# An attention product folded into two feed-forward layers in fp32: weight product in three fp32r passes, first loads regrouped, small tiles padded to 64 bytes

## What is computed

```python
qn = q / (norm(q, axis=1) + 1e-06)      # q, k, v: (1, 6016, 256)
kn = k / (norm(k, axis=1) + 1e-06)
s = kn.transpose(0, 2, 1) @ qn / tau    # (256, 256)
s = s - s.max(-1, keepdims=True)
a = exp(s); a /= a.sum(-1, keepdims=True) + 1e-09
x = v @ a
h = x @ w_in                            # (256, 2048)
x = (h - tanh(h)) @ w_out               # (2048, 256)
h = x @ w_in2
g = where(h > 0, h, exp(min(h, 0)) - 1)
out = g @ w_out2
```

## Time and profile before

| | |
|---|---|
| median of 3 runs (lowest, highest) | 1108.56 us (1108.1, 1110.02) |
| the profiled execution: its time, its span | 1108.33 us, 1106.5 us |
| PE busy | 1097.6 us, 99% of the span, 4892 matmul records |
| DVE, ACT, POOL busy | 703.6 (64%), 533.3 (48%), 0.8 us (0%) |
| chain that ended last | PE 98%, DVE 1%, DMA 1% |
| DMA | 33.42 MB; 344 and 333 GB/s in the first two of 40 slices, 1 to 20 in most later ones |

### The profile page before, as it was taken

How to read it: one execution, slowest core, us unless ns; L and a number is a source line. 1 busy time by engine, 2 the same in 40 slices (tenths; PEclk the granted TensorE clock), 3 DMA queues, 4 the chain that set the end, 5 groups by cost and what they waited for, 6 DMA issues and landing times.

```text
span 1106.5 us, 14123 instructions
## 1 busy us (share of the span) xinstructions
PE 1097.6 (99%) x4892; PEld 904.8 (82%) x4892; DVE 703.6 (64%) x1133; ACT 533.3 (48%) x891; POOL 0.8 (0%) x7
## 2 busy tenths in 40 slices
PE   8999999999999999999999999999999999999998
PEld 7768888888888888888888888888888888888998
DVE  5676666665665656666666666666565565666565
ACT  6565555444444544544544444444454444444443
POOL 0000000000000000000000000000000000000000
PEclk9999999999999999999999999999999999999999
DMA  9941010110101101001011011010110010001010
GB/s 344 333 112 20 1 20 1 20 19 1 20 1 20 19 0 19 12 7 19 0 19 19 0 19 19 0 19 3 16 19 0 14 19 0 0 4 16 1 20 15
DMA packets 105710, 33.42 MB, mean 30 GB/s; under 512 B 96849, under 2 KB 101841, under 8 KB 105169
## 3 DMA queue, kind: packets, MB, share of 16 engines
q1 hardware_dynamic: 105680, 33.04, 12.1%
HBM read 26.87 MB, written 6.16 MB: 30 GB/s over the span
## 4 chain that ended last, share of the span: by engine, by line
PE 98%; DVE 1%; DMA 1%; ACT 0%; SPq 0%; issue 0%; ACTq 0%
PE h_ps L356 16%; PE h_ps L358 15%; PE h_ps L357 15%; PE x_ps L358 8%; PE x_ps L356 8%; PE out_ps L358 8%; PE out_ps L356 8%; PE x_ps L357 8%; PE out_ps L357 8%; PE x_ps L364 3%; PE out_ps L414 1%; DMA q_ring<-q_dram 1%; PE h_ps L414 0%; PE x_ps L414 0%; DVE g_lo L675 0%; SPq L288 0%
## 5 line engine op out<-in xcount | busy, mean ns | idle before, releaser
L675 DVE TENSOR_TENSOR g_lo<-g,g_hi 128x512 fp32r<-128x512 f32 (+1 forms) x384 | 261.4, 681 | 225.3 <-ACT g_hi L616 116.8
L616 ACT ACTIVATE g_hi<-g 128x512 fp32r<-128x512 f32 (+1 forms) x192 | 119.6, 623 | 205.6 <-DVE g L793 205.2
L602 ACT ACTIVATE g_hi<-g 128x512 fp32r<-128x512 f32 (+1 forms) x192 | 119.6, 623 | 131.3 <-PE x_ps L358 70.5
L609 ACT ACTIVATE g<-h_ps 128x512 f32<-128x512 f32 (+1 forms) x192 | 113.1, 589 | 142.2 <-PE h_ps L358 141.4
L774 DVE TENSOR_TENSOR g<-h_ps,g 128x512 f32<-128x512 f32 (+1 forms) x192 | 129.6, 675 | 34.6 <-ACT g L595 34.5
L356 PE MATMUL h_ps<-x_hi,w_in_hi 128*128 128x512 f32 (+1 forms) x384 | 149.6, 390 | 0.1
L356 PE MATMUL h_ps<-vT_hi,wf_hi 128*128 128x512 f32 (+1 forms) x384 | 149.6, 390 | 0.0
L357 PE MATMUL h_ps<-vT_lo,wf_hi 128*128 128x512 f32 (+1 forms) x384 | 149.5, 389 | 0.0
L358 PE MATMUL h_ps<-x_hi,w_in_lo 128*128 128x512 f32 (+1 forms) x384 | 149.2, 389 | 0.0
L789 DVE TENSOR_SCALAR g<-g 128x512 f32<-128x512 f32 (+1 forms) x192 | 80.9, 421 | 107.4 <-ACT g L609 106.4
L358 PE MATMUL x_ps<-g_hi,w_out_lo 128*128 128x512 f32 (+1 forms) x384 | 149.0, 388 | 0.0
(11 more groups left out here) (90 smaller groups left out, 1080.3 us busy)
## 6 DMA issues: line engine op xcount, KB each, us to landing
v_blocks<-v_dram SPq DMA_DIRECT2D x88, 64.0 KB, 2.2
out_dram<-out_sb SPq DMA_DIRECT2D x88, 64.0 KB, 1.9
k_ring<-k_dram SPq DMA_DIRECT2D x9, 512.0 KB, 9.7
q_ring<-q_dram SPq DMA_DIRECT2D x9, 512.0 KB, 10.2
stage_a<-moe_w_in_dram SPq DMA_DIRECT2D x1, 2048.0 KB, 10.2
stage_b<-moe_w_out_dram SPq DMA_DIRECT2D x1, 2048.0 KB, 9.5
w_in_raw<-moe_w_in_dram SPq DMA_DIRECT2D x1, 2048.0 KB, 9.1
stage_a<-moe_w_out_dram SPq DMA_DIRECT2D x1, 2048.0 KB, 8.2
```

The source lines that it names most:

```text
L602: nc.scalar.activation(g1_hi[i % 2][:, 0:n], g1[i % 2][:, 0:n], ACT.Copy).then_inc(g1_rounded, 1)
L609: nc.scalar.activation(g2[i % 2][:, 0:n], h2_ps[i % 2][:, 0:n], ACT.Exp).then_inc(exp2_ready, 1)
L616: nc.scalar.activation(g2_hi[i % 2][:, 0:n], g2[i % 2][:, 0:n], ACT.Copy).then_inc(g2_rounded, 1)
L675: return nc.vector.tensor_tensor(lo, x, hi.bitcast(F32), ALU.subtract)
```

## The change

1. `CHUNKS` begins with 2, 2, 3 rows in place of 1, 1, 2, 3; there are 14 chunks in place of 15. `DIRECT` is 2. The q transfers of the first three chunks are issued by ACT, ahead of everything else on its queue; SP issues the k transfers and the rest. The load of tau moves behind the seventh chunk.
2. w_in is loaded in four transfers of 512 KB, one for each g. ACT rounds each into `w_in1_hi`, DVE forms the rest into `w_in1_lo`, in place over `stage_a`. `w_in1_hi` lies over the ring buffers that are last used by chunks 8 and 9. ACT writes `aT_hi` in place of `aT`, and DVE forms `aT_lo`. Each of the eight parts of the weight product is six fp32r matmuls (high-high, high-low, low-high, two each) in place of two plain fp32 ones.
3. The nine small tiles take 64 bytes each, so that all tiles start on multiples of 64.

```diff
-CHUNKS = [1, 1, 2, 3] + [4] * 9 + [2, 2]
+CHUNKS = [2, 2, 3] + [4] * 9 + [2, 2]
-DIRECT = 3
+DIRECT = 2
+Q_BESIDE = 3
 TAIL = 4
+FREED_FIRST = [i % RING for i in (LAST - TAIL - 1, LAST - TAIL)]
+ALIGNED = 16
...
-        stage_a = sb("stage_a", [P, CC * F])
+        with ExitStack() as early:
+            stage_a = sb("stage_a", [P, CC * F], stack=early)
+        w_in1_lo = sb("w_in1_lo", [P, GROUPS, CC, 512], F32R)
...
-        aT = sb("aT", [P, CC, C])
-        tau_sb, inv_tau = sb("tau_sb", [P, 1]), sb("inv_tau", [P, 1])
...
+        aT_hi, aT_lo = sb("aT_hi", [P, CC, C], F32R), sb("aT_lo", [P, CC, C], F32R)
+        def column(name, n):
+            return sb(name, [P, ALIGNED])[:, 0:n]
+        tau_sb, inv_tau = column("tau_sb", 1), column("inv_tau", 1)
...
         with ExitStack() as early:
-            k_ring = [sb(f"k_ring{i}", [P, CH, C], stack=early) for i in range(RING)]
...
+            k_ring = {i: sb(f"k_ring{i}", [P, CH, C], stack=early) for i in FREED_FIRST}
...
         with ExitStack() as early:
+            w_in1_hi = sb("w_in1_hi", [P, GROUPS, CC, 512], F32R, stack=early)
...
                 for ring, rows_of, loaded in ((k_ring, k_rows, loaded_k), (q_ring, q_rows, loaded_q)):
-                    sp.dma_start(ring[i % RING][:, 0:rows, :],
-                                 rows_of[:, ROW0[i]:ROW0[i] + rows, :]).then_inc(loaded[i % RING], 16)
-                if i == 0:
+                    if ring is k_ring or i >= Q_BESIDE:
+                        sp.dma_start(ring[i % RING][:, 0:rows, :],
+                                     rows_of[:, ROW0[i]:ROW0[i] + rows, :]).then_inc(loaded[i % RING], 16)
+                if i == RING:
                     sp.dma_start(tau_sb[:, :], tau.rearrange("(a b) -> a b", a=1).to_broadcast([P, 1])).then_inc(loaded_tau, 16)
-            sp.dma_start(stage_a[:, :].rearrange("p (a f) -> p a f", a=CC),
-                         w_in1.rearrange("(a p) f -> p a f", p=P)).then_inc(loaded_w_in1, 16)
+            w_in1_rows = w_in1.rearrange("(a p) f -> p a f", p=P)
+            for g in range(GROUPS):
+                sp.dma_start(stage_a[:, g * CC * 512:(g + 1) * CC * 512].rearrange("p (a f) -> p a f", a=CC),
+                             w_in1_rows[:, :, g * 512:(g + 1) * 512]).then_inc(loaded_w_in1[g], 16)
...
             for n, (g, m) in enumerate(WF_ORDER):
+                rows = slice(m * P, (m + 1) * P)
                 pe.wait_ge(aT_ready[m], 1)
+                pe.wait_ge(w_in1_rounded, g + 1)
                 if n in (4, 5):
                     pe.wait_ge(wf_split, n - 3)
                 for d in range(CC):
-                    last = nc.tensor.matmul(wf_ps[n][:, :], aT[:, d, m * P:(m + 1) * P],
-                                            w_in1_sb[:, d, g * 512:(g + 1) * 512], start=d == 0, stop=d == CC - 1)
+                    nc.tensor.matmul(wf_ps[n][:, :], aT_hi[:, d, rows], w_in1_hi[:, g, d, :], start=d == 0, stop=False)
+                pe.wait_ge(w_in1_split, g + 1)
+                for d in range(CC):
+                    nc.tensor.matmul(wf_ps[n][:, :], aT_hi[:, d, rows], w_in1_lo[:, g, d, :], start=False, stop=False)
+                pe.wait_ge(aT_split[m], 1)
+                for d in range(CC):
+                    last = nc.tensor.matmul(wf_ps[n][:, :], aT_lo[:, d, rows], w_in1_hi[:, g, d, :], start=False, stop=d == CC - 1)
                 last.then_inc(wf_multiplied, 1)
...
         @block.scalar
         def _(act):
+            q_rows = q[0].rearrange("(p r) c -> p r c", p=P)
+            for i in range(Q_BESIDE):
+                act.dma_start(q_ring[i][:, 0:CHUNKS[i], :], q_rows[:, ROW0[i]:ROW0[i] + CHUNKS[i], :]).then_inc(loaded_q[i], 16)
             act.wait_ge(ones_ready, 1)
...
+            def round_w_in1(g):
+                act.wait_ge(loaded_w_in1[g], 16)
+                if g == 0:
+                    act.wait_ge(chunk_multiplied, LAST - TAIL + 1)
+                nc.scalar.activation(w_in1_hi[:, g, :, :], stage_a[:, g * CC * 512:(g + 1) * CC * 512].rearrange("p (a f) -> p a f", a=CC),
+                                     ACT.Copy).then_inc(w_in1_rounded, 1)
+            for g in range(GROUPS - 1):
+                round_w_in1(g)
             act.wait_ge(norms_ready, 1)
             nc.scalar.activation(root[:, :], norms_ps[:, 0:2 * CC], ACT.Sqrt).then_inc(rooted, 1)
             nc.scalar.activation(table_warm[:, 1:2], ones[:, 0:1], ACT.Exp)
+            round_w_in1(GROUPS - 1)
...
-                nc.scalar.activation(aT[:, :, m * P:(m + 1) * P], aT_ps[m][:, 0:C].rearrange("p (d c) -> p d c", d=CC),
+                nc.scalar.activation(aT_hi[:, :, m * P:(m + 1) * P], aT_ps[m][:, 0:C].rearrange("p (d c) -> p d c", d=CC),
                                      ACT.Copy).then_inc(aT_ready[m], 1)
...
+            def split_w_in1(g):
+                dve.wait_ge(w_in1_rounded, g + 1)
+                minus(w_in1_lo[:, g, :, :], stage_a[:, g * CC * 512:(g + 1) * CC * 512].rearrange("p (a f) -> p a f", a=CC),
+                      w_in1_hi[:, g, :, :]).then_inc(w_in1_split, 1)
...
             norm_steps = [0]
+            split_w_in1(0)
             dve.wait_ge(rooted, 1)
...
             norm_step(nc.vector.tensor_scalar(rk[:, :], inv_norm[:, CC:2 * CC], inv_tau[:, 0:1], None, ALU.mult))
+            split_w_in1(1)
             dve.wait_ge(rq_ready, 1)
             for m in range(CC):
+                if m == 1:
+                    split_w_in1(2)
                 dve.wait_ge(scores_ready, m + 1)
...
+            def split_aT(m):
+                dve.wait_ge(aT_ready[m], 1)
+                rows = slice(m * P, (m + 1) * P)
+                minus(aT_lo[:, :, rows], aT_ps[m][:, 0:C].rearrange("p (d c) -> p d c", d=CC), aT_hi[:, :, rows]).then_inc(aT_split[m], 1)
+            split_aT(0)
+            split_w_in1(3)
             for m in range(CC):
                 dve.wait_ge(exp_ready, m + 1)
...
             for cc in range(CC):
                 transpose_v(0, cc)
+            split_aT(1)
             split_wf(0)
```

More of the change, by code:

```diff
@@ L118, in attention_ffn_kernel @@
         g1_lo = [sb(f"g1_lo{i}", [P, TILE], F32R) for i in range(2)]
-        stage_a = sb("stage_a", [P, CC * F])
+        with ExitStack() as early:
+            stage_a = sb("stage_a", [P, CC * F], stack=early)
+        w_in1_lo = sb("w_in1_lo", [P, GROUPS, CC, 512], F32R)
         ident = sb("ident", [P, P])
         ones = sb("ones", [P, P])
-        aT = sb("aT", [P, CC, C])
-        tau_sb, inv_tau = sb("tau_sb", [P, 1]), sb("inv_tau", [P, 1])
[L124 to L128, removed]
-        with ExitStack() as early:
-            k_ring = [sb(f"k_ring{i}", [P, CH, C], stack=early) for i in range(RING)]
-            q_ring = [sb(f"q_ring{i}", [P, CH, C], stack=early) for i in range(RING)]
+        aT_hi, aT_lo = sb("aT_hi", [P, CC, C], F32R), sb("aT_lo", [P, CC, C], F32R)
+        def column(name, n):
+            return sb(name, [P, ALIGNED])[:, 0:n]
+        tau_sb, inv_tau = column("tau_sb", 1), column("inv_tau", 1)
+        root, inv_norm = column("root", 2 * CC), column("inv_norm", 2 * CC)
+        rk = column("rk", CC)
+        table_warm = column("table_warm", 2)
+        neg_max = column("neg_max", CC)
+        row_sum, inv_sum = column("row_sum", CC), column("inv_sum", CC)
+        with ExitStack() as early:
+            k_ring = {i: sb(f"k_ring{i}", [P, CH, C], stack=early) for i in FREED_FIRST}
+            q_ring = {i: sb(f"q_ring{i}", [P, CH, C], stack=early) for i in FREED_FIRST}
+            for i in range(RING):
+                if i not in FREED_FIRST:
+                    k_ring[i] = sb(f"k_ring{i}", [P, CH, C], stack=early)
+                    q_ring[i] = sb(f"q_ring{i}", [P, CH, C], stack=early)
             k_sq, q_sq = sb("k_sq", [P, CH, C], stack=early), sb("q_sq", [P, CH, C], stack=early)
@@ L165, in attention_ffn_kernel @@
         loaded_q = [sem(f"loaded_q{i}") for i in range(RING)]
-        loaded_tau, loaded_v, loaded_w_in1 = sem("loaded_tau"), sem("loaded_v"), sem("loaded_w_in1")
+        loaded_tau, loaded_v = sem("loaded_tau"), sem("loaded_v")
+        loaded_w_in1 = [sem(f"loaded_w_in1_{g}") for g in range(GROUPS)]
+        w_in1_rounded, w_in1_split = sem("w_in1_rounded"), sem("w_in1_split")
+        aT_split = [sem(f"aT_split{m}") for m in range(CC)]
         loaded_w = {n: sem(f"loaded_{n}") for n in SPLIT_ORDER}
@@ L403, in _ @@
             transpose_prob(0)
-            w_in1_sb = stage_a[:, :].rearrange("p (a f) -> p a f", a=CC)
-            pe.wait_ge(loaded_w_in1, 16)
             for n, (g, m) in enumerate(WF_ORDER):
+                rows = slice(m * P, (m + 1) * P)
                 pe.wait_ge(aT_ready[m], 1)
+                pe.wait_ge(w_in1_rounded, g + 1)
                 if n in (4, 5):
```

## The result

The changed kernel takes 1103.92 us (median of 5 runs, 1103.7 to 1104.6) against 1108.56 before (five runs by then, with the same median as the three): a ratio of 0.9961, with 95% interval 0.995 to 0.9972. That is 4.6 us faster, above the 0.2% that such a measurement can tell. The forecast was 1105.2 in a range of 1102.4 to 1107.4. Run again beside later experiments it took 1104.33, against 1108.83 for the kernel before on that chip: ratio 0.9958 (0.9944 to 0.9971).

What follows compares the result with a forecast made beforehand. PE was taken to bound the kernel almost throughout from 10.79 us. Start 0.5 plus weight product 2.7 less DVE 0.1, with ACT and alignment at zero, gave 3.1 us: 1108.33 to 1105.2, range 1102.4 to 1107.4.

Steps and rivals of the forecast that it cites:

- What bounds the kernel: Whole kernel: from 10.79 us on PE works almost without a break; only the time before belongs to the q transfers.
- The start, -0.5 us: First loads and scores: larger first chunks and q issued by ACT gain 0.5 us, ends -0.2 and 1.2.
- PE starts at 4.3 to 4.4: First chunk of 2 rows: its data are in at 4.2 us, so PE begins 0.4 us later than before.
- If the rate doubles at 9.4 again: PE's clock during the first scores: doubling at 9.4 us puts row 4 at 10.3 instead of 10.79, gaining 0.5 us.
- The weight product, -2.7: Weight product on PE: 48 fp32r matmuls, 11.0 us, replace 16 fp32 ones, 13.7 us; gain 2.7, ends 2.5 and 3.4.
- ACT's new work, 0: Four roundings of 1.06 us each on ACT fit into its idle gaps around the square root, so they cost zero.
- the third near 40.5: Third of four w_in transfers, served in turn 1.3 us apart: lands near 40.5 us, rounded by 41.6, before the root.
- The second rival: The four w_in transfers mix and all end at 42; root 2.8 us late, 2.3 lost, 1107.5 us; chance 0.08.
- DVE, 0.1 given back: DVE's new differences in the weight product make it as tight as PE: 0.1 us lost, ends 0 and 1.0.
- Alignment, 0 with ends of 2.3: Main loop, 4656 matmuls: 64-byte starts change nothing, ends -2.3 and +2.3 us, since compared tiles took 393 and 394 ns.
- the clock and alignment case: PE's clock rises sooner or the main loop gains from alignment: 1 to 2.3 us more, 1103.4 us; chance 0.17.
- The slower rival: Main loop: moved tile addresses slow each matmul, 1.2 ns or more making the kernel over 0.2% slower, e.g. 1112.2; chance 0.05.

## Why the prediction was right, point by point

- **What bounds the kernel**: right. PE has 99% of the span in every run, and each gain was a pause, a rate or a piece of work of PE's.
- **The start, -0.5 us**: wrong in the profile (+0.47), and worth nothing by the medians. "PE starts at 4.3 to 4.4" was 4.79: I let k and q of chunk 0 have all of DMA, but six transfers on two queues share it. "If the rate doubles at 9.4 again" was the larger miss: it came at 10.9, and over eleven profiles between 9.1 and 13.2, more than twice as wide as the ends I had set (8.0 and 9.8) and mostly beyond them. One profile cannot give that term a value. The 500 ns between executions that the Trainium skill gives (TensorE: Matmul & The Clock Gate, Part 1) were too narrow here: in the four profiles with the new start, in which PE made no pause, the doubling came 4.2 to 6.1 us after its first record.
- **The weight product, -2.7**: right, 2.58 measured. 48 passes took 11.4 us without the transposes, 0.237 each in place of the 0.229 of the sum. It ended at 62.27, not near 61.2. The prediction had named a short product with a loop later than 61.5 as a sign against its DVE term; that sign came, but from the late start (product begun at 50.66 in place of 49.78) and the slower passes.
- **ACT's new work, 0**: right in sum, with less cover than I gave it. The third piece of w_in was rounded from 42.56 on, 2 us later than "the third near 40.5"; the root followed at once. Had the start gained what I forecast, this wait would have eaten part of it. The second rival, w_in landing as a whole, did not come: the roundings that waited for it began at 39.49, 40.85 and 42.56.
- **DVE, 0.1 given back**: right in size. From the end of the product to unit 2 PE took 2.77 us against 2.81, and the chain now runs through ACT and DVE there (wf_hi, wf_lo, w_out_lo, g). DVE's last idle time before that g is 0.58 us at 58.85, so by my estimate a still shorter product would have bought little; no run tried it.
- **Alignment, 0 with ends of 2.3**: the mechanism that I dismissed. It gave 1.6 us. The step that failed is the comparison of tiles at 64 with tiles 32 off, 393 and 394 ns: each of the two groups has weights and moving operands that start alike, so it could not show what a difference between them costs. The loss was largest at the handovers between them, two of 24 steps in a unit. The durations of single records could not show it; the distance between the starts of successive ones could.
- **The rivals**: the clock and alignment case at 1103.4 is nearest to what came, by its second half: the loop gained and the clock did not rise sooner. The slower rival did not come, but its mechanism exists: other addresses alone cost 10 to 11 us in two experiments, 2.1 and 2.3 ns a matmul against the 1.2 from which it was to be seen.

By the profiles the forecast's 3.1 us and the measured 3.8 differ by these terms: the start 0.97 less, the product 0.12 less, DVE 0.14 and the softmax 0.09 more, the loop 1.56 more. By the medians the gain is 4.6, and what is left over lies within the scatter of the start. That the total came so near is in part luck: the terms that were counted gave 2.5 us without alignment (1108.38 to 1105.91), and the one that was put at zero made up for the start.

## What to carry to other kernels

Where weight loads run beside matmuls, give all the tiles that PE reads the same start modulo 64 bytes, and pad small tiles so that a later allocation cannot part them: half-aligned cost 1% here, more than this whole change won. Read PE's rate from the distance between starts, group by group and at the handovers, not from durations. Before shortening the way to a wait, ask which engine becomes the bound at it, and keep ready work for PE to do there, since in one execution a pause of 1.5 us was followed by 3.4 us at half rate.

## What the runs showed of the hardware that I had not expected

- The second layer's weights and moving operands 32 bytes apart modulo 64: 11 and 12 us more over 4656 matmuls (1048.85 and 1049.96 against 1037.7), while all tiles off by 32 cost nothing (1037.71).
- TensorE's rate doubled anywhere from 9.1 to 10.9 us in four profiles with the same start and no pause, from 9.2 to 13.2 in seven with the old start, and fell to half after a pause of 1.51 us in one execution.
- From 4 to 10 us DMA moved 412 to 416 GB/s with q's first transfers on ACT's queue and 356, in one profile, with the same transfers on SP's alone.
